# Transposing probabilities in row halves, TensorE by fours, low parts on GpSimd, row sums by pairs of blocks

## What is computed

```python
scores = q @ k.T / sqrt(64) - slopes[h] * dist
scores = where(is_global | is_local, scores, -1e9)      # 8 global keys, 96 local ones
a = exp(scores - max(scores)); a = a / (sum(a) + 1e-9)
x = (a @ v) as [1536, 512]
h = x @ w_in; g = (a0 + a1*h + a2*h^2 + a3*h^3) / (1 + |b0|*|h| + |b1|*h^2 + 1e-6)   # d_ff 2048
x = g @ w_out
h = x @ w2_in; s = h * softmax(h)                                                    # d_ff 1024
out = layernorm(s) * g_ln @ w2_out
```

## Time and profile before

| | |
|---|---|
| median of 3 runs | 491.23 us |
| profiled execution: time, span | 491.82 us, 489.9 us |
| TensorE clock granted, mean | 0.999 |
| PE busy | 480.8 us (98%) |
| DVE busy | 380.6 us (78%) |
| ACT busy | 262.9 us (54%) |
| POOL busy | 63.0 us (13%) |
| chain that ended last, by engine | PE 86%, DVE 11%, ACT 2% |

### The profile page before, as it was taken

How to read it: one execution, slowest core, us unless ns; L and a number is a source line. 1 busy time by engine, 2 the same in 40 slices (tenths; PEclk the granted TensorE clock), 3 DMA queues, 4 the chain that set the end, 5 groups by cost and what they waited for, 6 DMA issues and landing times.

```text
span 489.9 us, 7177 instructions
## 1 busy us (share of the span) xinstructions
PE 480.8 (98%) x2560; PEld 390.8 (80%) x2560; DVE 380.6 (78%) x705; ACT 262.9 (54%) x474; POOL 63.0 (13%) x133
## 2 busy tenths in 40 slices
PE   7999999999999999999999999999999999999997
PEld 5777667888888887888888788888888888888885
DVE  5899996899999789888878999999785554554450
ACT  4999895655454556544545655444444333433341
POOL 4767765200000000000000000000000000000000
PEclk9999999999999999999999999999999999999999
DMA  8699969600000000000032336332012222222201
GB/s 289 212 400 416 406 233 373 223 34 0 1 0 1 1 0 1 0 1 0 1 87 86 113 102 193 88 110 84 0 44 64 66 65 64 64 64 64 73 34 43
DMA packets 26959, 50.22 MB, mean 103 GB/s; under 512 B 2224, under 2 KB 16560, under 8 KB 25392
## 3 DMA queue, kind: packets, MB, share of 16 engines
q1 hardware_dynamic: 23760, 37.23, 21.9%
q0 software_dynamic: 2880, 12.58, 7.6%
q10 hardware_dynamic: 288, 0.01, 0.0%
HBM read 40.38 MB, written 3.15 MB: 89 GB/s over the span
## 4 chain that ended last, share of the span: by engine, by line
PE 86%; DVE 11%; ACT 2%; issue 1%; POOL 0%; POOLq 0%; DVEq 0%
PE ps L1102 9%; PE ps L1104 9%; PE ps L1103 9%; PE ps L1032 8%; PE ps L1033 8%; PE ps L1034 8%; PE ps L1167 4%; PE ps L1165 4%; PE ps L1122 4%; PE ps L1166 4%; PE ps L1121 4%; PE ps L1120 4%; DVE negs L653 3%; PE ps L1148 2%; DVE bank_a_lo L690 2%; PE ps L963 2%
## 5 line engine op out<-in xcount | busy, mean ns | idle before, releaser
L1102 PE MATMUL ps<-gate_hi,bank_b_hi 128*128 128x512 f32 x192 | 74.8, 390 | 0.5 <-DVE tok_lo L852 0.5
L1032 PE MATMUL ps<-tok_hi,bank_a_hi 128*128 128x512 f32 x192 | 75.1, 391 | 0.0
L1033 PE MATMUL ps<-tok_lo,bank_a_hi 128*128 128x512 f32 x192 | 74.7, 389 | 0.0
L1034 PE MATMUL ps<-tok_hi,bank_a_lo 128*128 128x512 f32 x192 | 74.7, 389 | 0.0
L1103 PE MATMUL ps<-gate_lo,bank_b_hi 128*128 128x512 f32 x192 | 74.7, 389 | 0.0
L1104 PE MATMUL ps<-gate_hi,bank_b_lo 128*128 128x512 f32 x192 | 74.7, 389 | 0.0
L494 ACT ACTIVATE quad<-ps 128x1024 f32<-128x1024 f32 x24 | 24.7, 1029 | 69.9 <-DVE rest L794 67.0
L412 POOL TENSOR_SCALAR probs<-probs,small 128x256 f32<-128x256 f32 (+1 forms) x96 | 48.6, 519 | 24.7 <-DVE small L663 24.0
L452 ACT ACTIVATE probs<-negs,small 128x256 f32<-128x256 f32 (+1 forms) x96 | 46.1, 485 | 6.0 <-DVE small L653 5.7
L776 DVE SCALAR_TENSOR_TENSOR quad<-quad,small,absh 128x1024 f32<-128x1024 f32 x24 | 30.8, 1283 | 21.5 <-ACT absh L497 21.4
L497 ACT ACTIVATE absh<-ps,small 128x1024 f32<-128x1024 f32 x24 | 26.8, 1116 | 33.8 <-PE ps L1104 33.8
(11 more groups left out here) (94 smaller groups left out, 948.3 us busy)
## 6 DMA issues: line engine op xcount, KB each, us to landing
v_sb<-in_v_win SPq DMA_DIRECT2D x8, 704.0 KB, 7.6
bank_a_raw<-in_w_in SPq DMA_DIRECT2D x4, 1024.0 KB, 11.2
bank_a_hi<-in_w_in POOLq DMA_DIRECT2D x4, 1024.0 KB, 9.9
bank_b_raw<-in_w_out SPq DMA_DIRECT2D x4, 1024.0 KB, 9.8
bank_b_hi<-in_w_out POOLq DMA_DIRECT2D x8, 512.0 KB, 5.6
q_sb<-in_q_t SPq DMA_DIRECT2D x16, 192.0 KB, 5.9
k_sb<-in_k_win SPq DMA_DIRECT2D x8, 384.0 KB, 7.2
stage_hi<-tok_hi SPq DMA_DIRECT2D x12, 256.0 KB, 2.7
```

The costliest lines, as they stand in the source:

```text
L1032: pe.matmul(banks(bank, 1), bank_a_hi[:, f, ws], x_hi, start=(k == 0), stop=False)
L1033: pe.matmul(banks(bank, 1), bank_a_hi[:, f, ws], x_lo, start=False, stop=False)
L1034: mm = pe.matmul(banks(bank, 1), bank_a_lo[:, f, ws], x_hi, start=False, stop=(k == KT - 1))
L1102: pe.matmul(banks(4 + k, 1), bank_b_hi[:, f, ws], g_hi, start=first, stop=False)
```

## The change

1. TensorE transposes the rows 0 to 63 and 64 to 127 of a block by separate instructions with 64 columns of the identity, the first half into bank 4, the second into bank 5; the two banks hold a pair of blocks. ACT copies bank 4 and DVE bank 5 of each pair. `probs_t` holds a pair of blocks in a buffer and moves to the second half of the raw w_out area; there are 6 `probs` buffers, not 5.
2. TensorE's order is by four blocks: turn n and n+1, scores of four, turn n+2 and n+3, values of the four before. up(0), the values of the last four, up(1), up(2).
3. Sums and reciprocals are made once for two blocks; ACT and DVE go by pairs.
4. Of the low parts of w_in, 6 stay on DVE (from n = 34), 10 go to GpSimd, as do all 8 of w_out. SP loads the second half of w_out after all values.
5. `outs_at(n)` gives the block whose out (ACT) and low part (DVE) are made in the pair n.

```diff
-    PB, TB = 5, 4
+    PB, TB = 6, 4
+    probs_t = [at(f"probs_t{i}", [P, 2, 2 * WIN], F32, B_LO + 16 * KB + i * 2 * SLICE) for i in range(TB)]
...
+    def turned_at(n, r, first):
+        return banks(4 + r, 1)[:, n % 2 * WIN + first * D:n % 2 * WIN + (first + 1) * D]
...
-    SETUP_STEPS, STEPS_PER_BLOCK = 4, 2
+    SETUP_STEPS, STEPS_PER_PAIR = 4, 2
-    SPLIT_FROM, CAST_FROM, CAST_EVERY = 16, 10, 6
+    EARLY_IN, SPLIT_FROM, CAST_FROM, CAST_EVERY = 6, 34, 14, 7
+
+    def outs_at(n):
+        return [m for m in range(2, DONE_B0 - 1, 3) if n == m // 4 * 4 + 8 + (2 if m % 4 == 3 else 0)] + \
+            [m for m in (DONE_B0 - 1,) if n == HEADS - 2]
```

SP:

```diff
-                if 1 <= k <= 4:
-                    load_w_in(k - 1)
-            load_w_out()
+                if 2 <= k <= 5:
+                    load_w_in(k - 2)
+            load_w_out(0, 2)
+            sp.wait_ge(values_ready, HEADS)
+            load_w_out(2, 4)
```

GpSimd:

```diff
-                pool.wait_ge(dve_step, n * STEPS_PER_BLOCK + SETUP_STEPS + 2)
+                pool.wait_ge(dve_step, n // 2 * STEPS_PER_PAIR + SETUP_STEPS + 2)
...
+        def split_in_low(f):
+            pool.wait_ge(in_loaded[f // 4], 16)
+            pool.wait_ge(in_hi_loaded[f // 4], 16)
+            pool.tensor_tensor(bank_a_lo[:, f, :], bank_a_raw[:, f, :], bank_a_hi[:, f, :].bitcast(F32),
+                               ALU.subtract).then_inc(in_lo_late, 1)
+
+        def split_out_low(j):
+            tiles = slice(2 * j, 2 * j + 2)
+            pool.wait_ge(outw_loaded[j // 2], 16)
+            pool.wait_ge(outw_hi_loaded[j], 16)
+            pool.tensor_tensor(bank_b_lo[:, tiles, :], bank_b_raw[:, tiles, :], bank_b_hi[:, tiles, :].bitcast(F32),
+                               ALU.subtract).then_inc(outw_lo_ready, 1)
+
+        for j in range(FT // 2):
+            split_out_low(j)
+            for f in (EARLY_IN + 2 * j, EARLY_IN + 2 * j + 1):
+                if f < FT:
+                    split_in_low(f)
```

ACT:

```diff
+            lo = 0 if n % BLOCKS else P
+            act.wait_ge(turned_ready, n + 2)
+            src = banks(4, 1)[:, lo:2 * WIN].rearrange("p (c q) -> p c q", q=D)
+            dst = probs_t[n // 2 % TB][:].rearrange("p u (c q) -> p (u c) q", q=P)[:, lo // D:, 0:D]
             act.activation(dst, src, ACT.Copy).then_inc(turned_copied_act, 1)
...
+        def attend_pair(n):
+            k = n + AHEAD
             if k < HEADS:
-                attend_exp(k, 0)
-            if n % 3 == 0 and 6 <= n < HEADS - 3:
-                attend_out(n - 4)
-            elif n == HEADS - AHEAD:
-                attend_out(DONE_B0 - 1)
+                for h in range(2):
+                    attend_exp(k, h)
             attend_copy(n)
             if k < HEADS:
-                attend_exp(k, 1)
+                for h in range(2):
+                    attend_exp(k + 1, h)
+            for m in outs_at(n):
+                attend_out(m)
```

DVE:

```diff
         def attend_sums(n):
-            dve.wait_ge(exp_ready, 2 * n + 2)
-            dve.tensor_scalar(psums_eps[n % PB], psums[n % PB], 1e-9, None, ALU.add).then_inc(dve_step, 1)
+            dve.wait_ge(exp_ready, 2 * n + 4)
+            dve.tensor_scalar(psums_eps[n // 2 % 3], psums[n // 2 % 3], 1e-9, None, ALU.add).then_inc(dve_step, 1)
...
+        def attend_pair(n):
             if n + SUMS_AHEAD < HEADS:
                 attend_sums(n + SUMS_AHEAD)
             if k < HEADS:
                 attend_shift(k, 0)
...
                 attend_shift(k, 1)
...
+                for h in range(2):
+                    attend_shift(k + 1, h)
             attend_copy(n)
...
+            for m_out in outs_at(n):
+                attend_low(m_out)
+            if n >= SPLIT_FROM and (n - SPLIT_FROM) // 2 < EARLY_IN:
+                split_in_low((n - SPLIT_FROM) // 2)
...
-            split_out_low(0)
             gate_poly(0)
...
-            if c == 0 and j + 1 < GROUPS:
-                split_out_low(j + 1)
-            elif c == CHUNKS - 1:
+            if c == CHUNKS - 1:
```

TensorE:

```diff
         def wait_copied(n):
+            pe.wait_ge(turned_copied_act, n // 2 + 1)
+            pe.wait_ge(turned_copied_dve, n // 2 + 1)
...
                 for half in range(0 if i else 1, 2):
-                    c = h * WIN + half * P
-                    mm = pe.transpose(banks(4 + n % 2, 1)[:, c:c + P], probs[n % PB][:, h, half * P:(half + 1) * P],
-                                      ident[:])
+                    for r in range(2):
+                        rows = slice(r * D, (r + 1) * D)
+                        mm = pe.transpose(turned_at(n, r, 2 * half + h), probs[n % PB][rows, h, half * P:(half + 1) * P],
+                                          ident[rows, rows])
...
+        def attend_four(n):
             for m in (n, n + 1):
                 attend_turn(m)
+            for m in range(n + SCORES_AHEAD, min(n + SCORES_AHEAD + 4, HEADS)):
+                attend_scores(m)
+            if n == HEADS - 4:
+                for m in range(n - 4, n):
+                    attend_values(m)
+            for m in (n + 2, n + 3):
+                attend_turn(m)
+            if 0 < n < HEADS - 4:
+                for m in range(n - 4, n):
+                    attend_values(m)
...
+            for n in range(0, HEADS, 4):
+                attend_four(n)
+            pe.wait_ge(shifted_ready, 2 * HEADS - 4)
+            up(0)
+            for n in range(HEADS - 4, HEADS):
                 attend_values(n)
+            pe.wait_ge(shifted_ready, 2 * HEADS)
+            up(1)
             up(2)
```

More of the change, by code:

```diff
@@ L86, in attention_feed_forwards @@
     w = WORK
-    PB, TB = 5, 4
+    PB, TB = 6, 4
     negs = [[at(f"negs{i}{h}", [P, WIN], F32, w + (2 * i + h) * KB) for h in range(2)] for i in range(2)]
     w += 4 * KB
[L90 to L93, removed]
+    probs = [at(f"probs{i}", [P, 2, WIN], F32, w + i * SLICE) for i in range(PB)]
+    w += PB * SLICE
+    probs_t = [at(f"probs_t{i}", [P, 2, 2 * WIN], F32, B_LO + 16 * KB + i * 2 * SLICE) for i in range(TB)]
     w = WORK + 22 * KB
@@ L119, in attention_feed_forwards @@
     negmax = [cols(2) for _ in range(2)]
-    psums = [cols(2) for _ in range(PB)]
-    psums_eps = [cols(2) for _ in range(PB)]
-    prec = [cols(2) for _ in range(PB)]
+    psums = [cols(4) for _ in range(PB // 2)]
+    psums_eps = [cols(4) for _ in range(PB // 2)]
+    prec = [cols(4) for _ in range(PB // 2)]
     stat = [cols(12) for _ in range(2)]
@@ L266, in load_w_in, with load_w_out @@
             sp.dma_start(bank_a_raw[:, 4 * i:4 * i + 4, :], w_in[:, 4 * i:4 * i + 4]).then_inc(in_loaded[i], 16)
-        def load_w_out():
-            for i in range(4):
+        def load_w_out(first, last):
+            for i in range(first, last):
                 sp.dma_start(bank_b_raw[:, 4 * i:4 * i + 4, :], w_out[:, 4 * i:4 * i + 4]).then_inc(outw_loaded[i], 16)
@@ L290, in _ @@
             sp.wait_ge(dve_step, SETUP_STEPS)
-            load_w_out()
+            load_w_out(0, 4)
             for b in range(B):
@@ L517, in _ @@
                     attend_exp(n, h)
-            for n in range(HEADS):
-                attend_unit(n)
+            for n in range(0, HEADS, 2):
+                attend_pair(n)
             attend_out(HEADS - 4)
@@ L699, in attend_unit @@
             if k < HEADS:
-                if pr and m < 2:
-                    dve.wait_ge(bias_ready, 4 * pr + 2 + 2 * m)
+                if pr and m == 0:
+                    dve.wait_ge(bias_ready, 4 * pr + 2)
                 attend_shift(k, 0)
@@ L711, in attend_unit @@
                     attend_bias(pr, 1, OF_WINDOW)
-                if m in (BLOCKS + 2, BLOCKS + 3) and pr + 1 < PAIRS:
-                    attend_bias(pr + 1, m - (BLOCKS + 2), OF_FIRST)
-            if n % 3 == 1 and 7 <= n < HEADS - 3:
-                attend_low(n - 5)
-            elif n == HEADS - AHEAD:
-                attend_low(DONE_B0 - 1)
-            attend_copy(n)
-            f, part = divmod(n - SPLIT_FROM, 2)
-            if part == 0 and 0 <= f < FT:
-                split_in_low(f)
+                    dve.wait_ge(bias_ready, 4 * pr + 4)
+                for h in range(2):
+                    attend_shift(k + 1, h)
+            attend_copy(n)
+            if k < HEADS and m == BLOCKS + 2 and pr + 1 < PAIRS:
+                for h in range(2):
+                    attend_bias(pr + 1, h, OF_FIRST)
+            for m_out in outs_at(n):
+                attend_low(m_out)
+            if n >= SPLIT_FROM and (n - SPLIT_FROM) // 2 < EARLY_IN:
+                split_in_low((n - SPLIT_FROM) // 2)
         def full_attention():
@@ L824, in _ @@
             for n in range(2):
-                attend_sums(n)
+                dve.wait_ge(exp_ready, 2 * n + 2)
+                if n == 1:
+                    attend_sums(0)
                 attend_shift(n + 2, 0)
-                attend_reciprocals(n)
+                if n == 1:
+                    attend_reciprocals(0)
                 attend_shift(n + 2, 1)
-            for n in range(HEADS):
```

(5 more changed lines are left out.)

71 lines of the change are left out of this document (19 added, 52 removed).

## The result

The kernel changed takes 546.1 us, median of four executions (545.9 to 546.3, and one of 2666 us that no profile covers and that stays unexplained), against 491.35 us for the kernel before on the same chip. The ratio is 1.1116, 95% interval 1.1094 to 1.1138. The profiled execution has a span of 544.4 us, 54.5 more than before. The forecast said slower, at 519, range 499 to 531: the sign was right, the size too small by 27 us.

What follows compares the result with a forecast made beforehand. Prediction: ACT and DVE waiting for each other bound the attention, late gates the feed-forward; 491.8 + 12.8 (attention) + 14.6 (low parts on GpSimd) = 519.2, called 519 us, range 499 to 531.

Steps and rivals of the forecast that it cites:

- which two edits cost: Sums and outs by pairs in the attention, +12.8 us; late low parts on GpSimd in the feed-forward, +14.6 us.
- The loop of a pair with a low part: Attention: ACT and DVE releasing each other take 3.12 us a pair, 3.97 where a low part waits for its out.
- ACT's wait for the shifts: Attention: ACT idle in front of exps until DVE's shift, about 22 times 0.5 to 1.4 us, 22 us in all.
- The wait of the low part for its out: Attention: DVE's low part waits for ACT's out of the same pair, 0.85 us in 12 pairs, 10.2 us.
- The half transposes: TensorE in the attention: row halves running side by side save 0.43 us a pair; one behind the other, 0.9 dearer.
- SP's late half of w_out: Load that waits for all values, lands some 10 us on and is first wanted at group 4: costs nothing.
- So each waits for the other's whole operation and they alternate.: First feed-forward gates: DVE and GpSimd take turns operation by operation, stalling TensorE 4.6, 5.9 and 4.1 us, +14.6.
- TensorE's order "at nothing": Attention: TensorE by fours needs 1.1 to 1.3 us a block under a cover of 1.75, so it costs nothing.
- the ring: Attention: ACT's exps and out and DVE's low part, sums and shifts wait for each other; last sums start at 89.0.
- the sum had 3.97 less 0.35 for the first block: Attention: a pair with a low part takes 3.97 us, less 0.35 in the 7 pairs with a first block.
- the sum had 4.2: End of attention: from the last sums at 89.0, scalings, transposes, copy, out and low part bring up(0) at 93.2.
- Rival d: Whole kernel: TensorE idle in attention, clock grant falls to 1.2 GHz, 16 us more at worst, 535; chance 0.11.

Runs made afterwards that it cites:

- experiment 3: The kernel changed, only that ACT makes a pair's attend_out ahead of the pair's exps instead of behind them: 533.41 us.
- experiment 8: The kernel changed with outs ahead of exps, a shift ahead of sums, late low parts on DVE, and TensorE by twos instead of fours: 492.18 us.
- number 10: Kernel of experiment 8 with ten w_in low parts on GpSimd inside the attention and the first w_out low part ahead of gate 0: 498.50 us.
- number 11: Kernel of number 10 with up(0) after iteration 44 and up(1) after iteration 46 instead of after the attention loop: 495.23 us.

## Why the prediction was wrong

**Right.** The sign, and which two edits cost. The loop of a pair with a low part: 3.97 us forecast, 3.91 to 4.10 measured in seven of the twelve; ACT's wait for the shifts 22 us forecast, 21.3 measured, 24 times. The wait of the low part for its out: 10.2 forecast, 12.5 by experiment 3, in which TensorE's waits shrink as well. The half transposes: 0.43 us a pair saved forecast, 1.02 - 0.59 = 0.43 seen. SP's late half of w_out: nothing, no wait names it.

**The failed step, and most of the miss (16 us): "So each waits for the other's whole operation and they alternate."** It rested on the earlier trace rows, in which two scalings met one low part of DVE. There GpSimd had only two instructions in a row, and a wait ahead of them, so the rows could not tell "it gives way after each" from "it gives way when it stops". Eighteen subtracts with no wait between them that held kept DVE out for 31 us; with a wait for the end of the one before (experiment 2) they alternated at once. The stall was 30.6, not 14.6; with the alternation forced the stalls were 11.2, and with the slow matmuls behind them 17.3. The lengths of the subtracts were nearly right: 2.36 and 1.28 us on the average where I took 2.0 and 1.15, and the estimate from the Trainium skill (GPSIMD Engine Reference, Elementwise), 2.2, was nearer for the larger one. The Trainium skill (SBUF — State Buffer, Who interferes with whom) calls the sharing an exclusive lock, and the trace agrees; what the trace adds is that DVE did not get in between GpSimd's instructions.

**The second failed step (6.6 us): TensorE's order "at nothing".** "TensorE would need 1.1 to 1.3 us a block" counted its work and left out its waits. By fours, the values of block n - 4 stand behind outs and low parts that the same ring makes late; the row `PE ps L1018 <- DVE tok_lo L706` says 11.8 us in 8 times. up(0) began at 99.77, not 93.2. The timelines of the kernel changed show where the 6.6 us arise:

```profile
67.80 1.12 PE L1018 MATMUL ps<-probs_t,v_sb 128*64 128x128 f32 x8 [2.61 <-DVE tok_lo L706]
...
70.00 0.60 ACT L491 ACTIVATE probs_t<-ps 128x512 f32<-128x512 f32 x1 [1.01 <-PE ps L1000]
...
92.12 0.16 DVE L686 TENSOR_SCALAR small<-small 128x4 f32<-128x4 f32 x1
...
92.59 1.83 POOL L422 TENSOR_SCALAR probs<-probs,small 128x256 f32<-128x256 f32 x4 [2.48 <-DVE small L690]
...
97.22 0.71 PE L1000 MATMUL ps<-ident,probs 64*128 64x64 f32 x16
```

3.1 us are in the ring: its last sums start at 92.12, not 89.0. Most of them lie in two pairs, of 4.51 us (45.21 to 49.72) and 4.97 (67.56 to 72.53), where the sum had 3.97 less 0.35 for the first block. In the second, values wait 2.61 us for tok_lo, the transposes stand behind them, and ACT's copy waits 1.01 us for these, inside the ring. The other 3.5 us come behind the last sums: 7.65 us to up(0), where the sum had 4.2. The last scalings end at 94.42, but the last transposes start at 97.22, because TensorE's order has the values of four blocks in front of them (93.85, 3.44 us, of which about half is the clock). Experiment 3 takes TensorE's wait for tok_lo from 11.8 to 3.7 us, and experiment 8 prices fours against twos, with the places of the outs, at 3.7 us of the mark.

**The third (about 1.8 at the mark, 1.9 behind the stall): the clock.** Rival d was 0.11 and came in part. The grant was 0.86 from 48 to 72 us and 0.62 from 84 to 96, a mixture of 2.4 and 1.2 GHz, and 0.50, that is 1.2 GHz, while TensorE stood. up(0) took 4.5 us from first matmul to the values (99.77 to 104.28), not 2.75. I had discarded it in the sum because the earlier trace rows show 1.00; they are rows of a full TensorE. The Trainium skill says that transposes don't count as busy for the gate (TensorE: Matmul & The Clock Gate, Part 4); no run bears that out as the cause here, since number 8 makes the same transposes at 1.00 from 48 to 72 us. TensorE's idle share alone doesn't order the rows either: 0.62 goes with the lowest share (7.60 us busy of 12), but from 24 to 48 us the kernel changed has 16.76 of 24 at 0.89, from 48 to 72 18.13 at 0.86, and experiment 3 has 16.18 at 0.96 there. What made the grant fall stays open.

What stays open: how much of the attention's 8.4 us beyond the forecast is clock and how much is wait, since the two may feed each other; and why number 10 ran at 0.86 where number 11 ran at 1.00 in a stretch that their edits don't touch.

## What to carry to other kernels

Work moved to GpSimd must not be a train: here a stream of SBUF to SBUF subtracts with no wait that held in between shut out a DVE operation with two SBUF inputs for as long as it lasted, and a semaphore wait for the end of the one before, which left gaps of about 0.1 us (118.14 to 118.22), turned one stall of 30.6 us into 11.2 in three. When two in-order engines release each other, draw the ring before counting the work: how many finished items lie between them was worth more here than what an instruction costs, and two changes of order gave back 19.8 us. The cheaper transposes were worth 1.5 us, and only once the order was mended.

## What was not expected of the hardware

- A DVE operation that had begun 0.15 us ahead of GpSimd's first subtract still ended after the eighteenth (115.50, 31.96 us). By these rows the one which is recorded as starting first does not keep the access; with a wait between the subtracts it was the same for one subtract (115.55, 3.68 us).
- The exclusion doesn't go by size: beside a subtract of GpSimd a 128x4 addition took 1.23 us instead of 0.16, while a 128x256 shift with an input in PSUM kept its 0.41. Nor does it go by SBUF alone: a 128x4 reciprocal from SBUF to SBUF kept its 0.17 (66.24 in number 11, beside the subtract of 65.90 to 67.17).
- The subtracts kept their pace while DVE waited: 1.28 us for 512 columns in the unbroken stream, 1.27 in number 11; with gaps 2.15, as the two then took turns. For 1024 columns it was 2.36 and 2.93.
